# A paired matmul on half the rows each: the last in-product of two layers' tiles, side by side

## The reference

```python
out = np.einsum('hk,bskhg->bshg', softmax(weight), x_unf)      # 7 taps

def layer1(x, w_in, w_out):                                    # w_in 192 x 2048
    h = x @ w_in
    g = h * np.clip(h + 3.0, 0.0, 6.0) / 6.0
    return g @ w_out                                           # w_out 2048 x 192

def layer2(x, w_in, w_out, a, b):
    h = x @ w_in
    P = a[0] + a[1] * h + a[2] * h**2 + a[3] * h**3
    Q = 1.0 + np.abs(b[0]) * np.abs(h) + np.abs(b[1]) * h**2
    return (P / (Q + 1e-06)) @ w_out
```

## Time and profile before

| | |
|---|---|
| timed runs, median (lowest to highest) | 1202.87 us (1202.79 to 1202.98), 3 runs |
| the profiled execution: its own time | 1202.42 us |
| its span, first to last instruction | 1200.3 us |
| busy PE / ACT / DVE / POOL | 1185.5 / 1168.2 / 1157.7 / 1072.2 us |
| granted TensorE clock | 0.999 of full speed |

### The profile page before, as it was taken

One profiled execution on the slowest core, in us unless ns is written; L12 is line 12 of the kernel. 1 busy time (PEld: TensorE's weight loads), 2 busy tenths in 40 slices (PEclk: granted clock), 3 DMA queues, 4 the chain that ended last, 5 costly groups with the idle time before them and its releaser, 6 DMA issues.

```text
span 1200.3 us, 18336 instructions
## 1 busy us (share of the span) xinstructions
PE 1185.5 (99%) x5145; PEld 962.9 (80%) x5145; DVE 1157.7 (96%) x1776; ACT 1168.2 (97%) x2235; POOL 1072.2 (89%) x829
## 2 busy tenths in 40 slices
PE   8999999999999999999999999999999999999988
PEld 6778888888888888888888888888888888888754
DVE  7899999999999999999999999999999999999898
ACT  8899999999999999999999999999999999999997
POOL 6889989999999989999899998999989999898875
PEclk9999999999999999999999999999999999999999
DMA  4400000000001000010000000000000000000010
GB/s 150 150 1 10 6 18 1 23 10 23 1 1 32 1 23 1 1 32 1 23 1 21 12 1 23 1 23 10 1 23 1 23 1 1 14 1 14 1 44 13
DMA packets 11317, 22.06 MB, mean 18 GB/s; under 512 B 1744, under 2 KB 3152, under 8 KB 11216
## 3 DMA queue, kind: packets, MB, share of 16 engines
q1 hardware_dynamic: 10928, 20.89, 5.9%
q10 hardware_dynamic: 288, 0.01, 0.0%
HBM read 14.60 MB, written 6.29 MB: 17 GB/s over the span
## 4 chain that ended last, share of the span: by engine, by line
PE 91%; ACT 4%; DVE 2%; issue 2%; POOL 0%; DMA 0%; ACTq 0%; DVEq 0%; POOLq 0%
PE h L359 45%; PE y0b_acc L376 5%; PE y0b_acc L377 5%; PE y0a_acc L371 5%; PE y0a_acc L373 5%; PE y0a_acc L372 5%; PE y1b_acc L377 4%; PE y1a_acc L373 4%; PE y1a_acc L371 4%; PE y1a_acc L372 4%; PE y1b_acc L376 4%; ACT rsq L524 0%; ACT g_hi L600 0%; ACT y0a_acc L536 0%; ACT num L491 0%
## 5 line engine op out<-in xcount | busy, mean ns | idle before, releaser
L520 POOL TENSOR_TENSOR den<-den,sqr 128x512 f32<-128x512 f32 x246 | 358.9, 1459 | 91.1 <-ACT den L497 90.1
L594 POOL TENSOR_TENSOR g_lo<-g,g_hi 128x512 fp32r<-128x512 f32 x246 | 321.7, 1308 | 5.3 <-ACT g_hi L600 5.3
L484 POOL TENSOR_TENSOR g_lo<-r,g_hi 128x512 fp32r<-128x512 f32 x235 | 306.9, 1306 | 5.5 <-ACT g_hi L600 3.6
L514 DVE SCALAR_TENSOR_TENSOR num<-num,coef,h 128x512 f32<-128x512 f32 x246 | 183.8, 747 | 8.3
L547 DVE SCALAR_TENSOR_TENSOR h<-num,coef,h 128x512 f32<-128x512 f32 x238 | 178.1, 748 | 0.2
L509 DVE TENSOR_TENSOR num<-num,h 128x512 f32<-128x512 f32 x246 | 167.8, 682 | 10.1 <-ACT num L491 3.9
L491 ACT ACTIVATE num<-h,coef 128x512 f32<-128x512 f32 x246 | 176.4, 717 | 0.2
L524 ACT ACTIVATE rsq<-den 128x512 f32<-128x512 f32 x246 | 159.0, 646 | 10.3 <-POOL den L520 7.2
L470 DVE SCALAR_TENSOR_TENSOR r<-r,h 128x512 f32<-128x512 f32 x235 | 160.7, 684 | 4.8 <-ACT r L463 3.7
L600 ACT ACTIVATE g_hi<-g 128x512 fp32r<-128x512 f32 x246 | 162.2, 659 | 2.4 <-DVE g L569 0.7
L540 DVE SCALAR_TENSOR_TENSOR den<-den,h 128x512 f32<-128x512 f32 x238 | 161.8, 680 | 0.6 <-ACT h L536 0.3
(11 more groups left out here) (177 smaller groups left out, 2995.9 us busy)
## 6 DMA issues: line engine op xcount, KB each, us to landing
stage_w<-w_pack SPq DMA_DIRECT2D x16, 448.0 KB, 3.3
raw_a<-x_a SPq DMA_DIRECT2D x16, 259.0 KB, 3.3
out<-y_a SPq DMA_DIRECT2D x16, 256.0 KB, 2.0
out<-y_b SPq DMA_DIRECT2D x16, 128.0 KB, 2.3
raw_b<-x_b SPq DMA_DIRECT2D x14, 129.5 KB, 2.7
r<-w_pack SPq DMA_DIRECT2D x4, 96.0 KB, 2.1
raw_b<-x_b SPq DMA_DIRECT2D x4, 65.5 KB, 4.7
y_a<-w_pack SPq DMA_DIRECT2D x2, 96.0 KB, 2.1
```

The lines of the kernel that those rows point to most:

```text
L484: eng.tensor_tensor(g1_lo[t % 2][:, :], gated(t)[:, :], f32(g1_hi[t % 2][:, :]), ALU.subtract).then_inc(S["g1lo"], 1)
L514: eng.scalar_tensor_tensor(out=n, in0=n, scalar=a1, in1=h2_of(t), op0=ALU.add, op1=ALU.mult).then_inc(S["num1"], 1)
L520: eng.tensor_tensor(den_of(t), den_of(t), sqr_of(t), ALU.add).then_inc(S["den_sum"], 1)
L594: eng.tensor_tensor(g2_lo[t % 2][:, :], g2[t % 2][:, :], f32(g2_hi[t % 2][:, :]), ALU.subtract).then_inc(S["g2lo"], 1)
```

## The change

In each of the 236 steps in which both layers have an in-product, the fifth matmul of each is taken out of its row of five. The four first matmuls of layer 1's tile are issued, then the four of layer 2's, and then two matmuls on 64 rows each, one right behind the other: layer 1's on rows 0 to 63 into its bank, layer 2's on rows 64 to 127 into its own bank. `h1_done` is raised by the first of the two, `h2_done` by the second. In the other steps nothing changes.

What is computed changes too. The 64-row matmul multiplies the low b weights by one part of the input alone. In layer 2 that is the high part, since its high part is now stored on rows 64 to 127 (and layer 1's out weights are stored with b ahead of a, so that y_b's high part comes out on those rows). In layer 1 the rows are 0 to 63 for every block; for even blocks that is the high part, for odd blocks the low part, so there the product of low b weights and the high part is left out.

```diff
+        if one and two and p < NT and s < NT:
+            beside1.add(p)
+            beside2[s] = p
...
+        OUT_A, OUT_B, OUT_RAW = (P, 0), (0, DA), (DB, 0)
...
+        def in_product_half(eng, l, t, psum):
+            k, f = divmod(t, NF)
+            half = slice(DB, P) if l else slice(0, DB)
+            return eng.matmul(psum, win_lo[l][half, (2 * f + 1) * P:(2 * f + 2) * P], xb_hl[l][k % 2][half, :],
+                              start=False, stop=True)
...
-            in_product(eng, 0, t, h1_of(t), split).then_inc(S["h1_done"], 1)
+            if t in beside1:
+                in_product(eng, 0, t, h1_of(t), split, range(4))
+            else:
+                in_product(eng, 0, t, h1_of(t), split).then_inc(S["h1_done"], 1)
...
-            in_product(eng, 1, t, h2_of(t), ("x2a_hi", "x2a_lo", "x2b_lo")).then_inc(S["h2_done"], 1)
+            needs = ("x2a_hi", "x2a_lo", "x2b_lo")
+            if t in beside2:
+                in_product(eng, 1, t, h2_of(t), needs, range(4))
+                in_product_half(eng, 0, beside2[t], h1_of(beside2[t])).then_inc(S["h1_done"], 1)
+                in_product_half(eng, 1, t, h2_of(t)).then_inc(S["h2_done"], 1)
+            else:
+                in_product(eng, 1, t, h2_of(t), needs).then_inc(S["h2_done"], 1)
...
-            round_hi(eng, xb_hl[1][k % 2][0:DB, :], yb_acc[0][0:DB, :]).then_inc(S["x2b_hi"], 1)
+            round_hi(eng, xb_hl[1][k % 2][DB:P, :], yb_acc[0][DB:P, :]).then_inc(S["x2b_hi"], 1)
...
-            eng.tensor_tensor(x2b_rest[DB:P, :], yb_acc[0][0:DB, :], f32(xb_hl[1][k % 2][0:DB, :]),
+            eng.tensor_tensor(x2b_rest[0:DB, :], yb_acc[0][DB:P, :], f32(xb_hl[1][k % 2][DB:P, :]),
...
-            eng.tensor_tensor(xb_hl[1][k % 2][DB:P, :], x2b_rest[DB:P, :], yb_acc[0][DB:P, :],
+            eng.tensor_tensor(xb_hl[1][k % 2][0:DB, :], x2b_rest[0:DB, :], yb_acc[0][0:DB, :],
```

More of the change, by code:

```diff
@@ L145, in build_program @@
     course, p, s = [], -1, -1
+    beside1, beside2 = set(), {}
     while s < NT + SUM2 - NF + 1:
@@ L367, in out_product @@
             first, last = f == 0, f == NF - 1
-            a_hi, b_hl, a_lo = w[:, c:c + DA], w[:, c + DA:c + DA + P], w[:, c + DA + P:c + WO]
+            a_hi, b_hl = w[:, c + OUT_A[l]:c + OUT_A[l] + DA], w[:, c + OUT_B[l]:c + OUT_B[l] + P]
+            a_lo = w[:, c + DA + P:c + WO]
             if first:
@@ L837, in w_out_hi @@
             _, _, wo, _, raw_out = w_views(c)
+            at = OUT_RAW[c // n_chunks]
             eng.wait_ge(d_w[c % W_STAGES], 16 * (c // W_STAGES + 1))
-            round_hi(eng, wo[:, :, 0:DA + DB], raw_out).then_inc(S["wo_hi"], 1)
+            round_hi(eng, wo[:, :, at:at + DA + DB], raw_out).then_inc(S["wo_hi"], 1)
         def w_in_lo(eng, c):
@@ L850, in w_out_lo @@
             eng.wait_ge(S["wo_hi"], c + 1)
-            minus(eng, wo[:, :, DA + P:WO], raw_out[:, :, 0:DA], f32(wo[:, :, 0:DA]))
-            minus(eng, wo[:, :, DA + DB:DA + P], raw_out[:, :, DA:DA + DB], f32(wo[:, :, DA:DA + DB])) \
+            l = c // n_chunks
+            a, raw_a0, b, b_lo, raw_b0 = ((P, DB, DB, 0, 0), (0, 0, DA, DA + DB, DA))[l]
+            minus(eng, wo[:, :, DA + P:WO], raw_out[:, :, raw_a0:raw_a0 + DA], f32(wo[:, :, a:a + DA]))
+            minus(eng, wo[:, :, b_lo:b_lo + DB], raw_out[:, :, raw_b0:raw_b0 + DB], f32(wo[:, :, b:b + DB])) \
                 .then_inc(S["w_out_done"], 1)
@@ L1107 @@
         o = w_out.reshape(nf, tile, d).transpose(1, 0, 2)
+        if not packs:
+            o = np.concatenate([o[:, :, da:], o[:, :, :da]], axis=2)
         inn = inn.reshape(128, nf // WCHUNK, -1)
```

## The result

The changed kernel takes 1259.41 us (median of 4 runs, 1259.35 to 1261.02), the kernel before 1202.85 us beside it (1202.79 to 1202.98): 1.0473 times as long, 95% interval 1.0455 to 1.0491. That is 56.6 us more, where 5.5 us less were forecast.

The account below looks back on a forecast made before the run. PE was taken to set the pace, ACT close behind. Gains of 4.8 us before 1080 us and 2.3 after, less 1.6 for the later `h1_done`, made -5.5: 1196.9 + 0.45 gives 1197.3 us, own range 1190 to 1202 (overall 1190 to 1219).

Parts of the forecast that it names:

- part (1): On PE, two 128-row matmuls per paired step become two adjacent 64-row ones; streaming together, the step is 4.307 us.
- the nearest row: Run's end at 1195 us, 128x128 to 128x64 matmuls about 0.23 us apart; taken to price the pair at 0.23 to 0.25 us.
- the text's own bounds: Pair's cost on PE: 0.227 us lowest, 0.34 with a late second load, 0.453 in turn; highest, steps of 4.63 or 4.85.
- PE empties round the pair: Rival: PE empties before and after the pair, 0.163 us each; step 4.63, 1238 us, with uncovered loads 1284; chance 0.11.
- no overlap: Rival: the two halves run one after the other, 0.453 us; step stays 4.533, longer loop costs 14 us, 1217; chance 0.12.
- ACT's own order: ACT's instruction order causes waits that a shorter PE step leaves; only 7.9 us of ACT's waits for PE can go.
- the waits for the sum: ACT's `rsq2` waits for POOL's `den_sum`, 18 us in 900 (63 times); claimed not to go away with a shorter PE step.
- The later `h1_done`: It comes after eight matmul distances, not four, 0.907 us later in the step; gives back 1.6 us at step 4.307.
- the loop through `gate1`: Layer 1's in-product to `relu1`, to `gate1`, back to the next in-product: 3.7 us a step, 2.8 before.
- Changes (3): Layer 2's b rows stored low part first, layer 1's out weights b before a; same instructions, claimed to cost nothing.
- The waits for `den_sum` stand: Sign of being right: ACT's waits for POOL's sum stay as before, 18 us in the 900 us window.
- What would show it wrong: Signs: second half 0.11 or 0.23 us late, next matmul 0.4 us or more behind, or middle steps well below 4.5 us.

Follow-up runs that it names:

- the order alone: Changed kernel with both fifth matmuls on 128 rows again, in the places of the halves: 1220.36 us, 1.0149 times the kernel before.
- the two runs: The changed kernel, 1259.41 us, and the same with the pair moved right behind layer 1's four matmuls so `h1_done` comes early again, 1249.64 us.

## Why the prediction was wrong

**The step that failed** is in part (1): "So a column-wise change costs under 0.02 us and doesn't stop the loading ahead. I take the low end, 0.23 to 0.25 us, as the nearest row." The first sentence held, and was measured again at about 0.015 us a step for a trip there and back. The second carried it over to a change of rows, where both halves of it fail: nothing streams for 0.09 us, and the weights are loaded only then, 0.11 us bare, each way. The pair's place costs 0.227 + 0.41 = 0.64 us, not 0.23 to 0.25. By the text's own bounds this was the case "PE empties round the pair", given a chance of 0.11. Its two prices were steps of 4.63 us (1238) and, with bare loads, 4.85 us (1284); the step came out at 4.74 and the time at 1259.4. The emptying was priced too high (0.163 from the length of a record, a gap of 0.09 measured) and the bare loads exactly (0.11). "The nearest row" was near only in being the one row with any change of shape; the upper bounds did hold the result.

The Trainium skill, page "TensorEngine Tiling (Array Packing)", section "Key Properties", says that a change of the tiling mode drains TensorE. The runs agree for 128 against 64 rows, 0.2 us each way. With 64-column weights no drain showed, but whether these change the mode is not shown. This was the rule against the change, and no row of before tested it for rows.

**The halves side by side** (no overlap had 0.12): right. Both start at 602.93, one half alone costs one distance more a step, and on equal rows they run one after the other. The Trainium skill, page "TensorE: Matmul & The Clock Gate", section "The mechanism", has matmuls on different row groups start about 4 ns apart; the shared start (602.93 both) agrees.

**ACT's own order bounds the gain** to some 5 us: right. With the fifth simply left out the kernel takes 1195.85 us and its step in the middle is 4.52, against 1197.3 and 4.51 forecast with the later `h1_done` in it. Leaving out one more matmul changes nothing. What in that order holds the pace was only partly right: the waits for the sum were taken for it, and without them the step shrank by a third of what that would give, because `rec2` then waits for DVE.

**The later `h1_done`** (+1.6 at a step of 4.307, 14 at 4.533, 35 at 4.63, 81 at 4.85): the sizes came close, the mechanism was wrong for the greater part. At 4.533 the order alone cost 17.7 us. At 4.74, halfway between 4.63 and 4.85, the list reads 58 us, of which 0.207 x 236 = 49 is the step itself and 9 the order; 9.8 was measured. But the rule has only the loop through `gate1` in it, and from start to start that loop cost PE some 5 us more than before in the first case and nothing more in the second. The rest stands at the block ends, which the prediction did not name, where PE waits for `g1lo` and for ACT's `y_a` (9.4 and 8.2 us more than before). That 9 agrees with 9.8 is luck. At the forecast's own step of 4.307 us it could not be tried, since nothing here makes the pair cost one distance.

**"Changes (3) cost nothing"**: nothing in the traces speaks against it, but no run tested them alone. The run with the order alone has them too, so whatever they cost is inside its 17.7 us.

**"The waits for `den_sum` stand"**: they stand at a shorter PE step (from start to start 20 us without the fifth, 18 before). In the changed kernel they are smaller, from start to start 12 us (57 times); as idle time, which hides short waits, they fall from 7.1 us in 20 times to 1.8 in 9. That fits the slack that ACT has there.

**What would show it wrong** named the sign that came: the matmul after the pair starting 0.4 us or more behind (603.36 after 602.93).

The account of the 56.6 us: (0.41 - 0.227) x 236 = 43 for the round trips, 0.025 x 236 = 6 for the wider distances behind the pair, and some 8 to 10 for the order (8.5 from start to start at the block ends, 9.8 between the two runs). What makes the distances behind the pair 0.230 and not 0.227 us is open.

## What to carry to other kernels

Count the trips between row shapes, not the matmuls. At 512 columns a trip from 128 to 64 rows and back costs 0.41 us here, and each pair side by side saves 0.22, so one pair a trip loses 0.2 us. An estimate from these two numbers: two pairs a trip would about break even, and only more in a row would gain; no run tried either against 128-row matmuls. Before pricing an operation by its nearest row, ask in what it differs from that row: here rows against columns was the whole matter, and a bound without a row against it deserved more than one chance in nine. And before making PE shorter, find the next engine's own pace from start to start: here even leaving out two matmuls was worth only 7 us. And when a size comes out as forecast, look whether it came by the way that was forecast: the order's 9 us did not.

## What the runs showed of the hardware

- A matmul on 64 rows and one on the other 64 rows, into different banks, start together (602.93 both); on the same rows they take one distance each (records at 603.37 and 603.70, of which 0.11 us is the first's load).
- Between 128x128 and 64x128 nothing streams for 0.09 us and then the weights load bare (0.11 us), each way, with a single half as with a pair. Inside the 64-row stretch loads run ahead as usual (601.39 for matmuls at 601.62).
- Between weights of 128x128 and of 128x64 loads run ahead, and the trip costs about 0.015 us (3.4 us in 220).
- A 64-row matmul of 512 columns takes as long as one on 128 rows (0.22 us for a second pair).
